# A fused attention and two-stage expert kernel on one core: first-layer matmuls two blocks ahead over three PSUM banks, weight halves and order arithmetic re-dealt between ScalarE, GpSimd and VectorE, and the last two row blocks in order

## The reference, cut to what matters

```python
attn_out = attention(q, k, v)          # B 2, H 8, S 768, D 64; local window of 96 keys plus 8 global keys
x = attn_out as (1536, 512)            # N 1536 tokens, width 512
# first expert stage: 8 experts, each token goes to its best one
expert_idx = argmax(xn @ en.T / tau)
for e in range(8):                     # w1[e] 512x1024, w2[e] 1024x512
    mask = expert_idx == e
    x1[mask] = gate_w[mask] * (relu(x[mask] @ w1[e]) @ w2[e])
# second stage: 4 experts, every token goes through all of them
p = domain_probs / sum(domain_probs)
for e in range(4):
    out += p[:, e] * (relu(x1 @ w1[e]) @ w2[e])
```

## Time and profile before

| | |
|---|---|
| time, median of 3 runs | 907.46 us (904.0 to 907.66) |
| the profiled execution's own time | 905.01 us |
| its span, first to last instruction | 903.2 us |
| TensorE busy | 844.7 us, 94% of the span |
| GpSimd, VectorE, ScalarE busy | 291.1, 287.8, 261.8 us |
| mean granted TensorE clock | 0.981 of full speed |

### The profile page before, as it was taken

One profiled execution on the slowest core, in us unless ns is written; L12 is line 12 of the kernel. 1 busy time (PEld: TensorE's weight loads), 2 busy tenths in 40 slices (PEclk: granted clock), 3 DMA queues, 4 the chain that ended last, 5 costly groups with the idle time before them and its releaser, 6 DMA issues.

```text
span 903.2 us, 13860 instructions
## 1 busy us (share of the span) xinstructions
PE 844.7 (94%) x4913; PEld 710.0 (79%) x4913; DVE 287.8 (32%) x797; ACT 261.8 (29%) x578; POOL 291.1 (32%) x161
## 2 busy tenths in 40 slices
PE   8999969766999999999999999999999999999996
PEld 5666659766999999878787878787878787878784
DVE  6877758851222231121212121212121212121211
ACT  5888855332545454111111111111111111111110
POOL 1520018573888887100164000164000065010101
PEclk9999979897999999999999999999999999999999
DMA  5776524326666666100033000033000000010101
GB/s 171 264 233 227 196 85 142 116 25 228 193 193 195 192 187 185 47 1 1 0 93 93 1 0 0 0 90 97 1 0 0 0 0 0 1 46 0 46 0 47
DMA packets 28024, 76.68 MB, mean 85 GB/s; under 512 B 6600, under 2 KB 6984, under 8 KB 27984
## 3 DMA queue, kind: packets, MB, share of 16 engines
q1 hardware_dynamic: 25584, 68.30, 24.5%
q0 software_dynamic: 2400, 7.87, 2.9%
HBM read 69.85 MB, written 6.30 MB: 84 GB/s over the span
## 4 chain that ended last, share of the span: by engine, by line
PE 86%; DVE 6%; DMA 2%; ACT 2%; issue 2%; SPq 1%; DVEq 0%; POOL 0%; ACTq 0%
PE ps L1368 29%; PE ps L1361 29%; PE ps L1325 9%; PE ps L1311 8%; PE ps L1205 3%; PE ps L1231 3%; PE ps L1217 3%; PE ps L1153 1%; DMA token_of<-tokd 1%; PE ps L1245 1%; DVE parts L1002 1%; DVE h L1121 1%; ACT h L634 1%; DMA win<-qkv 1%; PE ps L1300 1%
## 5 line engine op out<-in xcount | busy, mean ns | idle before, releaser
L1368 PE MATMUL ps<-ring,h 128*128 128x512 f32 x1152 | 276.4, 390 | 17.9 <-DVE h L1121 17.9
L1361 PE MATMUL ps<-x2T,ring 128*128 (+1 forms) x1152 | 275.0, 389 | 0.0
L1368 PEld LDWEIGHTS ps<-ring,h 128*128 128x128 f32 x1152 | 215.3, 188 | 67.4 <-DVE h L1121 23.0
L1361 PEld LDWEIGHTS ps<-x2T,ring 128*128 128x128 f32 x1152 | 216.1, 188 | 44.8
L279 POOL TENSOR_TENSOR ring<-raw,ring 128x1024 fp32r<-128x1024 f32 x96 | 230.4, 2408 | 61.0 <-ACT ring L587 57.5
L634 ACT ACTIVATE h<-ps 128x512 fp32r<-128x512 f32 x96 | 57.5, 599 | 476.6 <-PE ps L1361 476.6
L1121 DVE SCALAR_TENSOR_TENSOR h<-ps,h 128x512 fp32r<-128x512 f32 x96 | 66.4, 692 | 396.8 <-ACT h L634 396.8
L1325 PE MATMUL ps<-hT,ring 128*128 128x256 f32 x768 | 107.5, 291 | 21.2 <-DVE hT L1067 19.8
L500 POOL CAST ring<-raw 128x1024 fp32r<-128x1024 f32 x24 | 25.0, 1042 | 312.8 <-PE ps L1361 266.4
L1325 PEld LDWEIGHTS ps<-hT,ring 128*128 128x128 f32 x768 | 99.1, 196 | 23.7 <-DVE hT L1067 20.8
L1311 PE MATMUL ps<-x1T,ring 128*128 (+1 forms) x768 | 104.3, 286 | 1.7 <-DVE x1T L1062 1.7
(11 more groups left out here) (155 smaller groups left out, 424.2 us busy)
## 6 DMA issues: line engine op xcount, KB each, us to landing
raw<-wts SPq DMA_DIRECT2D x96, 512.0 KB, 3.9
win<-qkv SPq DMA_DIRECT2D x32, 320.0 KB, 3.1
win<-qkv SPq DMA_DIRECT2D x8, 384.0 KB, 4.5
x_rows<-xrow SPq DMA_DIRECT2D x12, 256.0 KB, 3.2
xrow<-consts SPq DMA_DIRECT2D x1, 768.0 KB, 4.5
xg<-x_rows,idx_now POOLq DMA_INDIRECT x14, 4.3
result<-acc,tokd POOLq DMA_INDIRECT x12, 2.7
idx_all<-token_of SPq DMA_DIRECT2D x10, 0.5 KB, 2.0
```

Of the source, the lines that this page charges most:

```text
L1361: ins = nc.tensor.matmul(ps[:, 4 + f % 2, :], w1(wp, f, k), x2T[:, xp * KD + k, bass.ds(g * 512, 512)], start=(k == 0 and n == 0), stop=(k ...
L1368: ins = nc.tensor.matmul(ps[:, t, :], h2[:, f % 2, hp_, t * P:t * P + P], w2(wp, f, 0, DM), start=(f == 0 and n == 0), stop=(f == KF - 1 a ...
```

## The change

- **Row blocks in order.** In `group`, the last two blocks f = 6 and 7 used to be projected together, row block by row block, after waiting for both. Now each f is projected by itself, as the others are.
- **First layer two blocks ahead, over three banks.** `hidden(p, f + 2)` stands ahead of `project(p, f)`, the two first blocks of a chunk run before its first `project`, and `h_bank(f)` spreads the blocks over banks 4, 5 and 2. `find_order` moves its result to bank 3.
- **Weight halves re-dealt.** GpSimd makes all eight quarters of the first expert during attention (six before), and SyncE loads all eight of the second during attention (six before). ScalarE makes no high half in the first chunk until f = 5; the rest follow in bunches, until chunk p = 0, f = 2.
- **Order arithmetic earlier.** The pieces on VectorE move one to two steps ahead, `gate_parts` and `pack(0)` from the second chunk into the first; one copy of `gate_parts` goes into attention; `find_order` stands at f = 3 instead of 5 of the second chunk, `gate_exps` at f = 4 instead of 5 of the first.
- **Late wait for further indices.** VectorE waits for `idx_more` from p = 5 on instead of from p = 1 on.
- Sixteen instead of 32 idle matmuls (`keep_busy`) stand ahead of the first expert stage.

```diff
+        def h_bank(f):
+            return (4, 5, 2)[f % 3]
...
-                if m % 2 == 0 and m and m // 2 < NQ + FILLED:
+                if m % 2 == 0 and m and m // 2 < 2 * NQ:
...
-            for c in range(1, 3):
-                for j in range(FILLED if c == 1 else 0, NQ):
-                    sp.wait_ge(split_done, NQ * (c - 1) + j + 1)
-                    load_quarter(sp, c, j, raw_ready)
+            for j in range(NQ):
+                sp.wait_ge(split_done, NQ + j + 1)
+                load_quarter(sp, 2, j, raw_ready)
...
-            for j in range(FILLED):
+            for j in range(NQ):
                 pool.wait_ge(raw_ready[j], 16)
                 nc.gpsimd.tensor_copy(ring[:, j, 0, :], raw[:, j, :]).then_inc(high_pool, 1)
...
-            lows(0, FILLED, NQ)
-            lows(1, 0, 4)
+            lows(0, 0, 4)
             pool.wait_ge(idx_next, 1)
-            lows(1, 4, 5)
+            lows(0, 4, 5)
             gather(idx_now)
-            lows(1, 5, FILLED)
+            lows(0, 5, NQ)
...
+            usual = [(), ((0, 6),), ((0, 7),), ((1, 0),), ((1, 1),), ((1, 2),), ((1, 3),), ((1, 4), (1, 5))]
+
+            def chunk(p, turns=usual, final=False, beside=None):
...
+                    for after, j in turns[f]:
+                        high_part(p + after, j, final and after)
...
-            chunk(-1, beside=(5, gate_exps))
+            chunk(-1, [(), (), (), (), (), ((1, 0),), ((1, 1), (1, 2)), ((1, 3), (1, 4))], beside=(4, gate_exps))
...
-            chunk(0)
+            chunk(0, [(), ((0, 5), (0, 6))] + usual[2:])
...
+                nc.vector.tensor_copy(parts[:, :, 0:2], origin)
...
             def gate_parts():
 
-                route(nc.vector.tensor_copy(parts[:, :, 0:2], origin))
...
-            chunk(-1, beside={1: [token_rounds], 2: [token_offsets], 3: [token_homes],
-                             4: [gate_logits], 5: [lambda: spot(lanes, 0, homes_ready, [0])], 6: [gates],
-                             7: [lambda: spot(lanes, 0, homes_ready, [1])]})
+            chunk(-1, beside={1: [token_rounds], 2: [token_offsets], 3: [token_homes, gate_logits],
+                              4: [lambda: spot(lanes, 0, homes_ready, [0])], 5: [gates],
+                              6: [gate_parts, lambda: spot(lanes, 0, homes_ready, [1])], 7: [lambda: pack(0)]})
...
-            chunk(0, beside={1: [gate_parts], 2: [lambda: pack(0)], 3: [lambda: pack(1)], 4: [number_extras],
-                             5: [choose_extras], 6: [read_order, read_extras], 7: [write_tables]})
+            chunk(0, beside={1: [lambda: pack(1)], 2: [number_extras], 3: [choose_extras], 5: [read_order],
+                             6: [read_extras], 7: [write_tables]})
...
-            with dve.Fori(1, prev) as p:
+            with dve.Fori(1, E - 3) as p:
                 hidden_part(p, 0)
                 y_low_part(p)
-                dve.wait_ge(idx_more, 16 * 2 * (CHUNKS - E))
+                chunk(p)
+            dve.wait_ge(idx_more, 16 * 2 * (CHUNKS - E))
+            with dve.Fori(E - 3, prev) as p:
+                hidden_part(p, 0)
+                y_low_part(p)
                 chunk(p)
...
             def chunk(p, final=False, beside=None):
+
+                hidden(p, 1)
                 for f in range(KF):
-                    if f + 1 < KF:
-                        hidden(p, f + 1)
-                    elif final:
-                        hidden2(0, 0, 0)
-                    else:
-                        hidden(p + 1, 0)
+                    if f + 2 < KF:
+                        hidden(p, f + 2)
+                    elif f + 1 == KF:
+                        if final:
+                            hidden2(0, 0, 0)
+                        else:
+                            hidden(p + 1, 0)
...
-                for f in range(KF - 2):
-                    hidden2(e, g, f + 1)
+                for f in range(KF):
+                    if f + 1 < KF:
+                        hidden2(e, g, f + 1)
                     may_project(f)
...
-            keep_busy(32)
+            keep_busy(16)
...
-            chunk(0, beside=(5, find_order))
+            chunk(0, beside=(3, find_order))
```

More of the change, by code:

```diff
@@ L454, in gather, with lows @@
                         in_offset=bass.IndirectOffsetOnAxis(ap=idx[:, h:h + 1], axis=0)).then_inc(gathered[h], 16)
-            def lows(c, first, end):
+            def lows(p, first, end):
                 for j in range(first, end):
-                    pool.wait_ge(high_act, c * NQ + (j - FILLED + 1))
+                    pool.wait_ge(high_act, p * NQ + (j + 1))
                     low_part(j, split_done)
@@ L475, in _ @@
             last = prev + 1
-            with pool.Fori(1, last) as c:
-                lows(c, FILLED, NQ)
-                lows(c + 1, 0, 4)
-                pool.wait_ge(idx_next, c + 1)
-                lows(c + 1, 4, 5)
+            with pool.Fori(1, last) as p:
+                lows(p, 0, 4)
+                pool.wait_ge(idx_next, p + 1)
+                lows(p, 4, 5)
                 gather(idx_now)
-                lows(c + 1, 5, FILLED)
+                lows(p, 5, NQ)
             for h in range(2):
                 pool.wait_ge(gathered[h], last * 16 + 32)
-            lows(last, FILLED, NQ)
             for j in range(NQ):
@@ L1042, in read_order @@
                 dve.wait_ge(homes_found, 1)
[L1043 removed]
+                got = ps[:, 3, 0:NT * 14].rearrange("p (r v) -> p r v", v=14)
                 nc.vector.memset(tokd[:, NT:], 0)
@@ L1310, in hidden @@
                     for n, (wp, xp) in enumerate(((0, 0), (0, 1), (1, 0))):
-                        ins = nc.tensor.matmul(ps[:, 4 + f % 2, 0:CH], w1(wp, f, k),
+                        ins = nc.tensor.matmul(ps[:, h_bank(f), 0:CH], w1(wp, f, k),
                                                x1T[:, xp * KD + k, bass.ds(((p + 1) & 1) * CH, CH)],
@@ L1333, in find_order @@
                 for t in range(NT):
-                    ins = nc.tensor.matmul(ps[:, 2, 0:NT * 14], lanes[:, t, :],
+                    ins = nc.tensor.matmul(ps[:, 3, 0:NT * 14], lanes[:, t, :],
                                            packs[:, t, :, :].rearrange("p r v -> p (r v)"),
@@ L1385, in group @@
                         ins = project2(e, g, f, t)
-                    ins.then_inc(hid_used, 1)
-                hidden2(e, g, KF - 1)
-                may_project(KF - 2)
-                may_project(KF - 1)
-                for t in range(4):
-                    ins = project2(e, g, KF - 2, t)
-                    if t == 3:
+                        if f == KF - 1:
+                            ins.then_inc(y2_ready, 1)
+                    if f < KF - 1:
                         ins.then_inc(hid_used, 1)
-                    project2(e, g, KF - 1, t).then_inc(y2_ready, 1)
-            keep_busy(32)
+            keep_busy(16)
             turn_x(-1, 0)
```

15 lines of the change are left out of this document (2 added, 13 removed).

## The result

The changed kernel takes 873.38 us (median of 4 runs, 872.75 to 874.66), the kernel before 906.98 (904.0 to 907.66, 4 runs): a ratio of 0.9638, 95% interval 0.9621 to 0.9654. The profiled execution took 874.66 us, its span 872.8 (before 905.01 and 903.2). The time lies in the range forecast (864 to 898), but 15.6 us from the forecast itself (889) and 1.4 us from rival 1 (872).

The account below looks back on a forecast made before the run. TensorE, busy 94% of the span, was taken as the bound, so gains come from its idle time. Terms -21.5 + 1.8 - 2.2 - 1.7 + 11.3 - 4.5 - 0.4 + 0.3 = -16.9 gave 889 us, range 864 to 898.

Parts of the forecast that it names:

- rival 1: First-stage chunks: VectorE gets one instruction in at each boundary between low halves; sum -32.8, 872 us; chance 0.21.
- Second stage, -21.5: In each group, `project2` of f = 6 behind `hidden2` of f = 7 removes 1.79 us, twelve times: -21.5 us.
- Tail, +1.8: At the span's end the stores queue on GpSimd, the last starting 3.1 us after the last matmul: +1.8 us.
- Seams, -2.2: Idling at each chunk's first `project` goes; chunks of 24.34 us become 23.9, for five chunks after the third: -2.2 us.
- Idle matmuls and attention, -1.4 together: Before the first stage: sixteen fewer idle matmuls, -1.7 us; two more quarters on GpSimd beside attention, +0.3 us.
- First chunk, +11.3: Four low halves shut out VectorE's index copy until 26.4; `project(-1, 6)` 9.3 us later, low clock 2.0: +11.3 us.
- Second chunk, -4.5: Six low halves shut out `number_extras` for 13.2 us; chunk 35.4 us against 39.9 before: -4.5 us.
- Third chunk, -0.4: The wait moves to ScalarE; four low halves shut out the index copy; 35.0 us against 35.4 before: -0.4 us.
- Rivals 3 and 4: 3: bunching continues in all five later chunks, 943 us, chance 0.06; 4: the group's wait stays, 909 us, chance 0.04.
- Rival 2: First-stage chunks: arithmetic not caught at all, since high halves come further apart; sum -42, 863 us; chance 0.17.

Follow-up runs that it names:

- the two last kernels: The changed kernel with all order arithmetic and the order's store early, without and with a pause behind the second chunk's gather: 861.53 and 860.08 us.
- cast last: Kernel before, with the origin copy moved from first to last of the five casts and subtractions of `gate_parts`: 906.64 us.
- arithmetic early: Changed kernel with all order arithmetic of the first chunk and the second pack at f = 1 to 4, `gate_exps` at f = 2: 874.52 us, ratio 0.9647.
- one step later: The "arithmetic early" kernel with `number_extras` and `choose_extras` one step later in the second chunk: 872.16 us.
- gather sooner: The "arithmetic early" kernel with GpSimd's second gather of the index copies' kind one low half sooner: 873.33 us.
- all early: Changed kernel with both chunks' arithmetic mostly in or ahead of the first chunk, and SyncE's store of the order between third-expert loads: 861.53 us, ratio 0.9514.
- gather ahead: Changed kernel with the gather for the third chunk's rows directly ahead of the first chunk's first low half: 879.49 us.
- pause: The "one step later" kernel with GpSimd waiting, behind the second chunk's gather, for a relu that comes 1.8 us later: 869.31 us.
- all early, pause: The "all early" kernel plus GpSimd's wait for a relu behind the second chunk's gather: 860.08 us, ratio 0.9508.

## Why the prediction was right or wrong

The time fell in the stated range because that range reached down past rival 1. The forecast's own account of the first two chunks did not hold; those of the second stage, the seams and SyncE's queue in the third chunk did.

**Second stage, -21.5: right.** The group is 43.52 us, and the part alone gives it in a kernel that is otherwise the one before. **Tail, +1.8:** measured +1.4. **Seams, -2.2:** measured -2.3; with one block ahead the later chunks are 24.35 again.

**Idle matmuls and attention, -1.4 together: measured -0.2.** Removing 16 of them gave 1.5 us where -1.7 was said, but they begin 1.3 us later (125.12, before 123.81 in the earlier trace rows) where +0.3 was taken. One meeting with a further quarter on GpSimd is seen, a tensor scalar at 60.42 that took 1.53 us where 0.43 stood before; the rest of that 1.3 was not traced. This pair of traces can't decide it: in the nine kernels whose program is the same up to here, the first `hidden` matmul starts anywhere from 129.5 to 131.7 us (median 131.1), and in the three with the attention of before from 131.9 to 132.6.

**First chunk, +11.3: the step that failed** is "VectorE reaches the copy of `next_indices` at about 18.1, and is shut out until 26.4". The bunch of low halves came at 17.1 after the first matmul, as worked out (17.0), and the copy at 18.2. But the copy ended at the first boundary. What followed is rival 1's course: one instruction of the chain for each low half. +7.2 was measured, rival 1 had +8.0.

**Second chunk, -4.5: the same step failed again**, "`number_extras`, behind `hidden_part` of f = 2, is issued at 4.7 and shut out for 13.2 us". It took 1.84 us, and the chunk 27.0 us, rival 1's number, where 35.4 was forecast. It is the largest part of the miss, 8.4 us. The -4.5 itself was taken from 39.9 us for the chunk before, which was 36.5; what was too much there was too little in the third, so the sum of the two is right.

The forecast rested on one row, the cast of 9.50 us, and rightly said that it ended with the low halves of the earlier trace rows. Its mistake was to take what had led up to those low halves for unimportant. The kernel before has a gather that ends 0.02 us ahead of them:

```profile
158.98 0.95 POOL L452 DMA_INDIRECT xg<-x_rows,idx_now  x1 [0.30 <-issue]
```

The runs forecast for the changed kernel began after a pause. Rival 1, which had the copy of 1.38 us and L947 on its side, was given 0.21, since each of the two had met one low half alone. But the trace before also holds a run of three without a gap, behind a pause of 3.81 us, in its first chunk (GpSimd, then VectorE):

```profile
136.41 8.14 POOL L279 TENSOR_TENSOR ring<-raw,ring 128x1024 fp32r<-128x1024 f32 x3 [3.81 <-ACT ring L587]
```

```profile
138.72 1.16 DVE L970 TENSOR_TENSOR big<-big,off 128x576 f32<-128x576 f32 x1
...
142.22 2.37 DVE L979 TENSOR_TENSOR tok_i<-tok_f 128x12 int32<-128x12 f32 x1
```

The low halves start at 136.41, 139.29 and 142.17. L970, issued in the first, is done at 139.88, 0.6 us into the second and with the third still to come; L979, issued in the third, is done as that ends. This is a run of several low halves that let VectorE in, in the trace that the forecast was made from, and it speaks for rival 1. The pair of experiments, gather added and pause added, shows that what stands directly ahead of the run decides; rows sorted by that would have led to rival 1's forecast.

The rule of the Trainium skill that was weighed there (SBUF — State Buffer, "SBUF: two separate sides" and "Who interferes with whom": a lock for a whole instruction, and issue order decides) thus agrees with the changed kernel's first chunk, where the copy, the casts and the tensor ops that met a low half end at the next boundary. It does not hold behind a gather, where 9.5 to 15.3 us were measured.

**Third chunk, -0.4: the mechanism right, the size off.** The wait moved to ScalarE, 11.93 us, and the quarter was late by SyncE's queue; the reload moved ahead removed 7.4 us. The four low halves that were to shut out the index copy there did not, so TensorE idled 4.75 us instead of 9.1, and 33.2 us came out against 35.0. Rival 1 had this wait right (4.9), but not what stood around it (30.8 us in all): it left out the 1.56 us at the chunk's start, where ScalarE waits for the tables, and took 2.0 for the slower matmuls behind the wait, which cost about 2.6.

**Rivals 3 and 4** are excluded: chunks four to seven take 23.9 us each, and the groups' wait is gone. Rival 2 did not come, since thirteen VectorE instructions of the first two chunks were held for over 1 us, but its time of 863 is about what the two last kernels reach by moving the arithmetic and the order's store.

## What to carry to other kernels

Before a long instruction in a trace is used as the price of a meeting of two engines, look at what the other engine did directly ahead of it, and look for short ones of the same kind: where both lengths stand in one trace, the difference between them is the thing to forecast. On GpSimd, don't let a run of SBUF operations start right behind an indirect DMA if VectorE has short copies, casts or tensor ops on SBUF operands then; a pause of 1.8 us was enough here. And when two engines wait side by side for one queue, taking one wait away is worth only the difference (2.9 us here); the queue's order is worth the whole (7.4).

## What the runs showed that was not expected

Short copies, casts and tensor ops of VectorE with one or two SBUF operands (no reductions or reciprocals) against runs of low halves on GpSimd, which start 2.34 us apart where VectorE is kept out, with what lies between the run and what GpSimd did before it:

| kernel | run starts, behind what | low halves | VectorE issued | took, us |
|---|---|---|---|---|
| before | 0.02 us behind a gather | 4 | 0.10 before the run | 9.50 |
| cast last | 0.02 behind a gather | 4 | 0.36 before | 9.78 |
| arithmetic early | 0.02 behind a gather | 6 | 0.07 before | 14.44 |
| one step later | 0.01 behind a gather | 7 | 2.09 in it | 14.67 |
| gather sooner | 0.02 behind a gather | 7 | 1.43 in it | 15.30 |
| all early | 0.02 behind a gather | 5 | 2.34 in it | 9.58 |
| gather ahead | 0.03 behind a gather | 5 | 0.42 before | 12.05 |
| before, first chunk | 3.81 us pause | 3 | 2.31 in it | 1.16 |
| changed | 16.39 pause | 5 | 1.07 in it | 1.36 |
| changed | 4.14 pause | 7 | 1.52 in it | 1.84 |
| pause | 1.82 pause | 8 | 0.29 in it | 2.45 |
| all early, pause | 2.05 pause | 8 | 0.30 in it | 2.33 |

Whether it was issued during the gather or in the first low half makes no difference. A gather by itself held nothing up here: where no low half follows directly, instructions issued 0.25, 0.50 and 0.79 us into one of 0.96 us took their usual 0.2 (changed kernel, 160.94, 161.19 and 125.53). Where a low half follows directly, even one alone, an instruction issued during the gather can be held with it: the changed kernel's cast L1048, issued at 189.65, 0.38 us into the gather of 189.27, took 3.02 us, to the end of the low half behind it, and casts of that size take 0.16 elsewhere. Why a gather directly ahead keeps VectorE out of all boundaries that follow stays open: the trace does not show who holds what between two GpSimd instructions, and no run had another kind of instruction than a gather ahead of such a run, nor a pause behind a gather shorter than 1.8 us. Behind a low half a shorter pause was enough: in the kernel with early arithmetic a run of four starts 0.92 us behind one, at 150.26, and the index copy issued at 151.27 took 1.44 us, to the first boundary.
